# q and k loaded with six neighbouring tokens per partition, and put in order by ScalarE's copies of their transposes

## The reference

```
q_d, k_d, v_d = means over each 4 neighbouring tokens       # 144 pooled tokens
out_up    = repeat(softmax(q_d k_d^T / 8) v_d, 4)           # each pooled row for 4 tokens
out_local = softmax(where(|i - j| < 4, q k^T / 8, -1e9)) v  # a band of 7 keys
x = out_up + out_local                                      # -> (2304 tokens, 512)
x = (sigmoid(x w_gate) * (x w_val)) w_out                   # feed-forward, 512 -> 1536 -> 512
out = soft mixture of 8 experts with 4 slots each (phi, w1, w2) over x
```

## Time and profile before

| | |
|---|---|
| median of 3 runs | 609.86 us (606.81 to 611.08) |
| profiled execution | 607.04 us, span 605.3 us |
| busy over the span | PE 554.4, PE weight loads 415.6, DVE 225.5, ACT 200.8, POOL 100.2 us |
| DMA | 70.97 MB, mean 117 GB/s |
| mean granted TensorE clock | 0.964 |
| chain that ended last | PE 84%, DMA 6%, DVE 4%, ACT 2%, issue 2% |

### The profile page before, as it was taken

How to read it: one execution, slowest core, us unless ns; L and a number is a source line. 1 busy time by engine, 2 the same in 40 slices (tenths; PEclk the granted TensorE clock), 3 DMA queues, 4 the chain that set the end, 5 groups by cost and what they waited for, 6 DMA issues and landing times.

```text
span 605.3 us, 11206 instructions
## 1 busy us (share of the span) xinstructions
PE 554.4 (92%) x4455; PEld 415.6 (69%) x4455; DVE 225.5 (37%) x504; ACT 200.8 (33%) x511; POOL 100.2 (17%) x171
## 2 busy tenths in 40 slices
PE   5687999999999999999999999999999999869963
PEld 4575777776777778777877877787777877624421
DVE  3495843425624252444234335432213112120213
ACT  4354654343343323252324333332222221211113
POOL 7554021132230202121111203010000000000000
PEclk9797799999999999999999999999999999978988
DMA  8879541212311111111020300003300307999958
GB/s 205 209 203 224 164 107 45 59 40 48 77 52 29 43 40 40 42 41 42 24 58 1 70 12 28 16 22 131 148 1 1 139 1 259 396 363 396 398 204 312
DMA packets 86708, 70.97 MB, mean 117 GB/s; under 512 B 61313, under 2 KB 65921, under 8 KB 86657
## 3 DMA queue, kind: packets, MB, share of 16 engines
q1 hardware_dynamic: 86656, 70.25, 37.5%
HBM read 65.52 MB, written 4.72 MB: 116 GB/s over the span
## 4 chain that ended last, share of the span: by engine, by line
PE 84%; DMA 6%; DVE 4%; ACT 2%; issue 2%; SPq 1%; DVEq 0%
PE gateb L897 26%; PE valb L897 25%; PE unitb L905 4%; PE unitb L854 3%; DMA ew_low<-in_moe_w_dram 3%; PE unitb L810 3%; PE unitb L926 2%; PE unitb L817 2%; PE unitb L845 2%; PE unitb L912 2%; PE unitb L972 2%; PE unitb L825 2%; DMA qtok<-in_q_dram 2%; PE unitb L832 2%; PE gateb L990 1%
## 5 line engine op out<-in xcount | busy, mean ns | idle before, releaser
L897 PE MATMUL gateb<-w_hl,xhl 128*128 128x512 f32 x648 | 162.8, 400 | 0.0
L897 PE MATMUL valb<-w_hl,xhl 128*128 128x512 f32 x648 | 161.5, 398 | 0.0
L897 PEld LDWEIGHTS gateb<-w_hl,xhl 128*128 128x128 f32 x648 | 119.0, 189 | 32.9 <-issue 8.7
L897 PEld LDWEIGHTS valb<-w_hl,xhl 128*128 128x128 f32 x648 | 117.9, 188 | 23.0
L628 ACT ACTIVATE hid<-gateb 128x512 f32<-128x512 f32 x54 | 32.3, 597 | 177.1 <-PE gateb L897 174.0
L744 DVE SCALAR_TENSOR_TENSOR hid<-hid,valb 128x512 f32<-128x512 f32 x54 | 37.1, 688 | 126.4 <-PE valb L897 126.3
L546 POOL TENSOR_TENSOR vd<-v 72x256 f32<-72x256 f32 x16 | 12.1, 756 | 173.2 <-PE unitb L838 168.3
L557 ACT ACTIVATE hT<-unitb 128x512 f32<-128x512 f32 x54 | 32.1, 594 | 13.2 <-PE unitb L905 12.9
L727 DVE TENSOR_TENSOR xraw<-unitb,outd 128x192 f32<-128x192 f32 x43 | 15.0, 355 | 56.2 <-PE unitb L854 56.0
L905 PE MATMUL unitb<-ident,hid 128*128 128x128 f32 x216 | 33.2, 276 | 1.1 <-DVE hid L744 0.4
L905 PEld LDWEIGHTS unitb<-ident,hid 128*128 128x128 f32 x216 | 25.0, 140 | 6.1 <-issue 2.3
(11 more groups left out here) (180 smaller groups left out, 665.6 us busy)
## 6 DMA issues: line engine op xcount, KB each, us to landing
ew_low<-in_moe_w_dram SPq DMA_DIRECT2D x19, 1024.0 KB, 14.3
ew_high<-in_moe_w_dram SPq DMA_DIRECT2D x13, 1024.0 KB, 13.5
qtok<-in_q_dram SPq DMA_DIRECT2D x32, 144.0 KB, 2.9
ktok<-in_k_dram SPq DMA_DIRECT2D x32, 144.0 KB, 3.2
v<-in_v_dram SPq DMA_DIRECT2D x32, 144.0 KB
out_dram<-outs SPq DMA_DIRECT2D x18, 256.0 KB, 3.0
vloc<-in_v_dram SPq DMA_DIRECT2D x32, 112.0 KB
xraw<-in_moe_w_out_dram SPq DMA_DIRECT2D x12, 256.0 KB, 3.7
```

Of the source, the lines that this page charges most:

```text
L897: last = mm(bank[:, :], xhl[:, i % NX, x, kk, :], w_hl[:, c, m, w, kk, :], start=j == 0, stop=j == len(order) - 1)
```

## The change

The source of the q and k loads is read with six neighbouring tokens for each partition (token = 6 x partition + tile) in place of 96 tokens per tile (token = 96 x tile + partition). Tile t then holds tokens t, t + 6, t + 12 and so on, and so does its transpose in PSUM. The copies into `qT` and `kT` write column n of tile t to position 6n + t, so both tensors hold what they held before. Everything that reads them is as it was.

```diff
             for h in range(2):
-                sp.dma_start(dst[:, :, h, :], src[b][2 * p + h].rearrange("(t p) d -> p t d", p=TT)).then_inc(s, 16)
+                sp.dma_start(dst[:, :, h, :], src[b][2 * p + h].rearrange("(p t) d -> p t d", p=TT)).then_inc(s, 16)
...
                 t0, t1 = TOKEN_TILES[int(name[1])]
-                copy(qT[:, t0 * TT:t1 * TT], ub[:, 0:(t1 - t0) * TT], SCALE_D).then_inc(free, 1)
+
+                copy(qT[:, :].rearrange("p (n t) -> p t n", t=NT)[:, t0:t1, :],
+                     ub[:, 0:(t1 - t0) * TT].rearrange("p (t n) -> p t n", n=TT), SCALE_D).then_inc(free, 1)
             elif name in ("K0", "K1"):
                 wait_unit(act, s)
                 wait(act, k_pooled, arg)
                 t0, t1 = TOKEN_TILES[int(name[1])]
-                copy(kT[:, t0 * TT:t1 * TT], ub[:, 0:(t1 - t0) * TT]).then_inc(free, 1)
+                copy(kT[:, :].rearrange("p (n t) -> p t n", t=NT)[:, t0:t1, :],
+                     ub[:, 0:(t1 - t0) * TT].rearrange("p (t n) -> p t n", n=TT)).then_inc(free, 1)
```

## The result

The changed kernel takes 611.12 us in the median of 20 runs (609.60 to 615.17), the kernel before 608.13 in 20 (606.44 to 611.08). The ratio is 1.0054, 95% interval 1.0035 to 1.0074: slower by 0.54%, about 3.3 us. The profiled execution took 609.67 us with a span of 607.9, 2.6 us more than that of before.

The account below looks back on a forecast made before the run. The prediction took TensorE to bound the body, and the head to hold about 20 us of its idle time, with DMA 0.87 busy. Loads 0 and copies 0 left 607.0 us as profiled, 609.9 at the median; range 605 to 616.

Parts of the forecast that it names:

- likeliest case: Whole kernel: loads 0 and copies 0, so no change, 609.9 us at the median; chance 0.60.
- Rival A: Copies into qT and kT double their column time: +2.2 us, 612 us at the median; chance 0.14.
- Packets unchanged: q and k loads: packets stay at 256 B, with 61,313 packets under 512 B again.
- Rival C: q and k loads: reads cover 1,536 B in larger packets, minus 2 to 4 us; chance 0.08.
- Cost of a packet and order in DRAM: q and k loads: about 9 ns is the packet's own cost, order in DRAM alone buys nothing; 0 us.
- No instruction is added: Whole change: no instruction, wait or transfer added, removed or moved past another, on any queue; SP issues the same loads.
- upper bound: Loads: neighbouring rows hinder one another, +4 us in all. Copies: column time doubles, 0.98 us per pair.
- The copies: ScalarE's stepped writes into qT and kT: no extra time, judged by GpSimd's stepped pooling reads; 0 us.
- What of it shows: Five head pairs, if copies double: fourth nearly all 0.98 us, three others 0.3 each at most; together +2.2 us.
- The body's cover: Body: ScalarE has 183 us without work in 280, hiding longer copies; without it eleven pairs would show 11 us.
- Rival B: Head: ScalarE's stepped write becomes the last wait ahead of S0, 616 to 622 us; chance 0.12.
- Rival D: Head: neighbouring reads also free the backlog's other transfers, -7 us, 603 us at the median; chance 0.06.

Follow-up runs that it names:

- long rows: Changed loads into a destination with one head's six rows on end, copies written four or two columns on end, heads mixed up, against the kernel before: 607.23 us, 0.9976.
- head loads: Kernel before with the new load order only for pairs 0 to 5, old order after that, copies of before: ratio 1.0011 (0.9986 to 1.0036).
- runs of four: Changed kernel with copies that read PSUM in steps of 384 B and write SBUF four or two columns on end: ratio 1.0032 against the kernel before.
- copies only: Kernel before with only the two stepped copies of the change, loads of before: 609.95 us, ratio 1.0025 (1.0004 to 1.0046).
- one load: As the long rows, but one load for both heads of a pair: 607.48 us, ratio 0.9983 against the kernel before.
- body again: The body loads kernel measured a second time, unchanged, against the kernel before: ratio 1.0002 (0.9979 to 1.0025).
- loads only: Kernel before with only the source order of the q and k loads changed: 610.98 us against 608.57, ratio 1.0032.
- body loads: Kernel before with the new load order only for pairs 6 to 15, copies of before: ratio 1.0028 (1.0009 to 1.0047).
- steps 3 and 8: Kernel before with q copies writing in steps of 3 columns and k copies of 8: 693 and 893 ns for 384 columns; no total time given.

## Why the prediction was right or wrong

- **The time.** 609.9 us was forecast and 611.12 came, inside 605 to 616, and within 1% of before, which had 0.82. That the two differ by only 1.2 us is luck: the kernel before has 608.13 in 20 executions, 1.7 us under the 609.86 of the three that I started from. The likeliest case said no change, and there is one: +0.54%, made of two terms that I had both put at zero. Rival A, copies that double at +2.2 us, has one of the two and is nearest to the truth.
- **Packets unchanged.** Right, to the count. The long rows show why: the shorter run cuts, on the destination side too. Rival C did not come. In the kernel that has such packets it brings about 1.5 us where 2 to 4 were named.
- **Cost of a packet and order in DRAM.** Nothing speaks against the zero: from 3.0 to 3.5 us the changed kernel moves 163 GB/s at a share of 0.71, so 230 for full engines where it was 223.

```profile
3.00:3.50 0.50, 0.00 (x0) 0.00 (x0) 0.00 (x0) 0.00 (x0) 0.50 (x1) 1.00 0.71 163
```

- **"No instruction is added" was taken to mean that SyncE's part costs the same.** This step failed. The DMA engines in the row above stand idle for 0.29 of the time, where they were full, while SyncE issues one load after the other, each 0.13 to 0.25 us longer. The loads alone cost about 2 us (1.0032; 1 to 1.5 by the head loads) where I had 0, within the +4 of the upper bound but by a mechanism that I had not named. I had read how long SP stood at a full queue and not what one issue takes. That the longer issue is the whole of the loads' cost is the reading that fits the traces; no run changed the issue alone.
- **The copies.** I took no extra time, since GpSimd's stepped reads cost none. That step failed: reads of another engine say nothing of ScalarE's writes. The upper bound came, and a little more: 876 and 573 ns where doubling gave 815 and 490. Columns went from 0.85 ns to (876 - 573) / 192 = 1.6, and two copies back to back from 0.71 to 1.20 us, which makes the 0.98 us per pair of the bound; ScalarE's 14.4 us more stand against 15.7.
- **What of it shows.** The bound said +2.2 us by the pairs of the head; it is 1.5 us by copies alone (1.0025) and about 1.3 by the changed kernel against runs of four (1.0054 against 1.0032). The traces have it pair by pair. The first pair was given 0.29 us. From the start of K0 (5.69 us) to the first scores the kernel before takes 2.00 us:

```profile
7.69 1.43 PE L817 MATMUL gateb<-kT,qT 64*64 64x70 f32 x20
```

  The changed kernel takes 2.29 (6.46 to 8.75), and so do the other three with stepped writes within 0.02; of the ten without, nine take 2.00 or 2.01, and the long rows, whose filler starts late, 2.31. The fourth pair was named as the place where nearly all 0.98 us shows. There the wait of the scores for kT rose from 0.25 us to 1.17, in the changed kernel and in copies only alike:

```profile
41.75 1.32 PE L820 MATMUL unitb<-kT,qT 64*64 64x70 f32 x36 [1.17 <-ACT kT L557]
```

  The third pair, given up to 0.3, shows nothing: from K0 to the scores it is 3.24 us before, after and in copies only. The other two have other waits. So 1.2 us can be pointed at where 2.2 was the sum, and the two pairs that were worked out in full came right. Copies only still starts its first feed-forward product at 65.2 us, like the kernel before, so a single trace doesn't show the 1.2 us at the end of the head. The body's cover held.
- **Rival B** would have needed 2.8 times the column time; 1.9 came. **Rival D** had nothing to it.

No run gives a version to put in the place of the kernel before. The long rows come nearest, at a ratio whose interval just reaches 1, but with the heads mixed up: their transposes read 128 neighbouring columns, and the two heads of a token are no longer neighbours. No run has a transpose that reads them as two pieces.

## What to carry to other kernels

A bound taken from a neighbour's row holds for that engine and for that side, read or write, alone: where a page names a penalty for an access and no row shows it, give it more weight than a row of another engine. When a destination order has to change, let the step fall on the PSUM side and keep at least two, better four, float32 columns on end on the SBUF side. And a load "with more on end in DRAM" gains only if the destination runs on as well: look at the shorter run, and at what one issue takes on the queue's engine. And before a difference of some 0.3% is believed, compare executions of like granted clock, and take a control of the kernel against itself.

## What the runs showed of the hardware that was not expected

- ScalarE, float32 from PSUM to SBUF, 384 columns: 490 ns on end, 522, 693, 875, 876 and 893 at steps of 8, 12, 16, 24 and 32 B; 506 ns when runs of four are written and PSUM is read with a step of 384 B. For 192 columns: 327 on end, 340 in runs of two.
- A load whose source runs on for 1,536 B while the destination is in pieces of 256 B takes at least 569 ns to issue on SyncE; 317 ns when both are in pieces or only the source is, 327 and 317 when both run on (long rows, one load).
- The last stage has two lengths in kernels with and without the change, taken as the rest of the span after the first transpose of `acc`. Where the three transposes take 273 ns in the median it is 68.5 to 68.9 us in eight traces (68.5 in those of before and after) and 70.6 in one, body again; where they take 418 to 421 ns it is 69.7 to 70.3 us in five (loads only, copies only, body loads, long rows, steps 3 and 8). The first row is of the kernel before, the second of loads only, ns min, median and max and first and last start:

```profile
L951 PE MATMUL unitb<-ident,acc x3: 272/273/299, 536.8 to 537.0; 128*128 128x128 f32 x3
```

```profile
L951 PE MATMUL unitb<-ident,acc x3: 421/421/444, 541.4 to 541.8; 128*128 128x128 f32 x3
```

In the stretches around them, columns as in the earlier trace rows, the granted clock is 1.00 (2.4 GHz) before and 0.50 (1.2 GHz) in loads only:

```profile
536.50:537.50 1.00, 0.52 (x3) 0.31 (x3) 0.61 (x2) 0.17 (x1) 0.00 (x0) 1.00 0.47 137
```

```profile
541.00:542.00 1.00, 0.61 (x3) 0.50 (x3) 0.73 (x2) 0.00 (x0) 0.00 (x0) 0.50 0.79 107
```

The three transposes themselves take 0.4 us more at the lower clock. Most of the rest lies later, and it holds for body again too. From 45 to 50 us after the first of them the granted clock is 0.90 to 0.94 in the eight traces with the short stage and 0.59 to 0.69 in the six with the long one. The kernel before, and body again:

```profile
581.80:586.80 5.00, 4.62 (x46) 1.86 (x40) 0.52 (x2) 0.38 (x1) 0.00 (x0) 0.91 0.23 84
```

```profile
581.20:586.20 5.00, 5.00 (x42) 1.79 (x34) 0.00 (x0) 0.38 (x1) 0.00 (x0) 0.59 0.27 99
```

What lowers the clock there, no run shows. This alone moves a single execution by 1.5 us, half of what the change cost, so no comparison of times here rests on one execution's total.
